# Expert weights split into high and low parts during the feed-forward stage, and the expert stage's activation low parts made on VectorE

## What is computed

```python
def _attn_ref(r, k, v, w, u):            # 4 batches, 8 heads, 768 steps, head size 48
    ...
        cur = np.einsum('bhd,bhe->bhde', u[None] * kt, vt)
        y[:, :, t] = np.einsum('bhd,bhde->bhe', rt, state + cur)
        state = w[None, :, :, None] * state + np.einsum('bhd,bhe->bhde', kt, vt)

def _moe_ref(x, w_in, w_out):            # x 3072 x 384, w_in 384 x 2048, w_out 2048 x 384
    h = x @ w_in
    g = h - np.tanh(h)
    return (g @ w_out).astype(np.float32)

def _moe2_ref(x, expert_emb, tau, w1, w2):   # 8 experts, w1 384 x 1024, w2 1024 x 384 each
    ...
    expert_idx = np.argmax(logits, axis=1)
    ...
        h = np.maximum(x[mask] @ w1[e], 0.0)
        out[mask] = gate_w[mask, None] * (h @ w2[e])
```

## Time and profile before

| | |
|---|---|
| median of 3 runs | 997.98 us (991.91 to 999.63) |
| the profiled execution | 993.31 us, of which the span of its instructions is 991.2 us |
| PE (TensorE matmul) | 918.6 us busy, 93% of the span |
| PEld (TensorE weight load) | 823.9 us, 83% |
| DVE (VectorE) | 623.7 us, 63% |
| ACT (ScalarE) | 476.8 us, 48% |
| POOL (GpSimd) | 380.1 us, 38% |
| granted TensorE clock, mean | 0.960 |

### The profile page before, as it was taken

The page is one execution under the profiler, slowest core; times in us unless marked ns, Lnnn a source line. Parts: engine busy times, 40 slices in busy tenths (PEclk is TensorE's granted clock), DMA queues, the critical chain, the costliest instruction groups (busy, mean ns, idle before and its releaser), DMA issues. The chain is left out here.

```text
span 991.2 us, 17791 instructions
## 1 busy us (share of the span) xinstructions
PE 918.6 (93%) x5314; PEld 823.9 (83%) x5315; DVE 623.7 (63%) x928; ACT 476.8 (48%) x1224; POOL 380.1 (38%) x369
## 2 busy tenths in 40 slices
PE   5999999999999999999999998787978979799995
PEld 4888887899999999999999988676967868689894
DVE  8799997998888788788888768844134041300000
ACT  3455445556556556656557452233424343254441
POOL 8689992000000000000000003777576575665652
PEclk7999999999999999999999997998989898899998
DMA  7698882001000000000000013754042231001100
GB/s 210 188 258 247 249 248 75 1 2 64 1 33 32 0 32 32 0 32 32 0 0 33 1 35 143 247 188 161 32 152 84 106 119 66 31 29 47 37 12 1
DMA packets 51766, 80.74 MB, mean 81 GB/s; under 512 B 6187, under 2 KB 36045, under 8 KB 51728
## 3 DMA queue, kind: packets, MB, share of 16 engines
q1 hardware_dynamic: 37776, 64.71, 20.9%
q0 software_dynamic: 3968, 10.82, 3.3%
q10 hardware_dynamic: 9984, 4.72, 1.7%
HBM read 66.07 MB, written 15.53 MB: 82 GB/s over the span
## 5 line engine op out<-in xcount | busy, mean ns | idle before, releaser
L1028 POOL MEMSET w_l<- 128x128 f32 x1 | 0.2, 204 | 435.5 <-POOLq L632 435.5
L751 ACT ACTIVATE usq<-h_ps 128x512 f32<-128x512 f32 x96 | 57.5, 599 | 163.1 <-PE h_ps L630 163.1
L628 PE MATMUL y_ps<-wout_h,g_h 128*128 128x384 f32 x384 | 129.6, 337 | 0.3 <-DVE g_l L850 0.3
L630 PE MATMUL y_ps<-wout_h,g_l 128*128 128x384 f32 x384 | 129.3, 337 | 0.0
L629 PE MATMUL y_ps<-wout_l,g_h 128*128 128x384 f32 x384 | 129.1, 336 | 0.0
L1278 DVE CAST w_h<-w_raw 128x3072 fp32r<-128x3072 f32 x14 | 34.9, 2491 | 138.9 <-PE e_bank L1350 134.2
L1321 POOL TENSOR_TENSOR ex_hT_l<-ex_hT,ex_hT_h 128x512 fp32r<-128x512 f32 x62 | 98.8, 1615 | 59.8 <-ACT ex_hT_h L1442 59.8
L1348 PE MATMUL e_bank<-w_h,ex_xT_h 128*128 x186 | 82.5, 444 | 39.5 <-POOL ex_xT_l L1311 35.6
L628 PE MATMUL h_ps<-xT_h,win_h 128*128 (+1 forms) x288 | 115.7, 402 | 0.8 <-DVE diff L843 0.8
L630 PE MATMUL h_ps<-xT_h,win_l 128*128 (+1 forms) x288 | 113.6, 394 | 0.0
L629 PE MATMUL h_ps<-xT_l,win_h 128*128 (+1 forms) x288 | 113.3, 394 | 0.0
(11 more groups left out here) (205 smaller groups left out, 2240.2 us busy)
## 6 DMA issues: line engine op xcount, KB each, us to landing
w_raw<-in_w SPq DMA_DIRECT2D x16, 1536.0 KB, 7.0
rT_sb<-in_rT SPq DMA_DIRECT2D x48, 96.0 KB, 2.6
kT_sb<-in_kT SPq DMA_DIRECT2D x48, 96.0 KB, 2.8
k_sb<-in_k SPq DMA_DIRECT2D x24, 192.0 KB, 2.9
r_sb<-in_r SPq DMA_DIRECT2D x24, 192.0 KB, 3.1
v_sb<-in_v SPq DMA_DIRECT2D x24, 192.0 KB, 3.5
x_dram<-xt_sb ACTq DMA_DIRECT2D x48, 96.0 KB, 3.2
xg_sb<-x_dram SPq DMA_DIRECT2D x6, 768.0 KB, 4.7
```

The costliest lines, as they stand in the source:

```text
L628: pe.matmul(out, lh, rh, start=start, stop=False)
L630: return pe.matmul(out, ll, rh, start=False, stop=stop)
L751: act.activation(usq[:, f % 2, :], h_ps[f % 2][:, :], ACT.Square).then_inc(u_done, 1)
```

## The change

The splitting of the expert weights leaves the expert stage. In every step of the feed-forward stage one piece of 128 x 512 of the 96 pieces of `w1` and `w2` is loaded (`load_piece`), its high part is made by ScalarE (`piece_high`, after `high`), its low part by GpSimd (`low` of the gpsimd block), and both are stored to two scratch tensors in DRAM, `w12_h` and `w12_l` (`store_piece`). The raw pieces have four buffers (`SPARE`), the parts two each (`MADE`). In the expert stage SyncE loads both parts of an expert straight into the slots, 6 MB in four transfers, and passes on that they have landed (`pass_turn`), after the transfers of turns 0 to 2 are issued. `w_raw` and all splits of it are gone. The low parts of the activations are now made by VectorE, which takes the transposed block from PSUM; ScalarE's plain copies `xT` and `hT` are gone, and so are GpSimd's subtractions. The host lays the raw weights out by piece.

```diff
@@ -637,14 +655,33 @@
                         sp.wait_ge(y_copied, B * g + b + 1)
                         sp.dma_start(x2_tiles[b, g], x2_sb[:, b, :]).then_inc(x2_stored, 16)
 
+                def load_piece(g, f):
+                    s = f % SPARE
+                    sp.dma_start(ew_raw[:, s, :], piece_of(w12, g, f)).then_inc(ew_loaded[s], 16)
+
+                def store_piece(g, f):
+                    s = f % MADE
+                    sp.wait_ge(ew_h_made, KF * g + f + 1)
+                    sp.dma_start(piece_of(w12_h, g, f), ew_h[:, s, :].bitcast(F32)).then_inc(ew_h_stored[s], 16)
+                    sp.wait_ge(ew_l_made, KF * g + f + 1)
+                    sp.dma_start(piece_of(w12_l, g, f), ew_l[:, s, :].bitcast(F32)).then_inc(ew_l_stored[s], 16)
+
                 def group(g, last):
                     if not last:
 
                         sp.wait_ge(xT_l_made, KD * g + KD)
                         load_group(sp, g + 1)
-                    if not isinstance(g, int) or last:
-                        store(g - 1)
-
+                    for f in range(KF):
+                        store_piece(g, f)
+                        if f + SPARE < KF:
+                            load_piece(g, f + SPARE)
+                        elif not last:
+                            load_piece(g + 1, f + SPARE - KF)
+                        if f == LAG and (not isinstance(g, int) or last):
+                            store(g - 1)
+
+                for f in range(SPARE):
+                    load_piece(0, f)
                 sp.dma_start(small[:, 0:1], tau.to_broadcast([P, 1])).then_inc(tau_in, 16)
 
...
@@ -652,6 +689,24 @@
                 groups(sp, group)
                 store(CH - 1)
                 sp.wait_ge(x2_stored, 16 * NT)
+                for i in range(MADE):
+                    sp.wait_ge(ew_h_stored[i], 16 * CH * KF // MADE)
+                    sp.wait_ge(ew_l_stored[i], 16 * CH * KF // MADE)
+
+            @block.gpsimd
+            def _(pool):
+                def low(g, f):
+                    s = f % MADE
+                    wait_apart(pool, passed_pool, (ew_h_made, KF * g + f + 1),
+                               (ew_l_stored[s], 16 * (KF // MADE * g + f // MADE)))
+                    pool.tensor_tensor(ew_l[:, s, :], ew_raw[:, f % SPARE, :], ew_h[:, s, :].bitcast(F32),
+                                       ALU.subtract).then_inc(ew_l_made, 1)
+
+                def group(g, last):
+                    for f in range(KF):
+                        low(g, f)
+
+                groups(pool, group)
 
             @block.tensor
...
@@ -762,6 +817,13 @@
                     wait(act, g_used, n - RING + 1)
                     act.activation(g_h[:, f % RING, :], poly[:, f % RING, :], ACT.Copy).then_inc(gh_done, 1)
 
+                def piece_high(g, f):
+                    s = f % MADE
+                    wait_apart(act, passed_x, (ew_loaded[f % SPARE], 16 * (TURNS * g + f // SPARE + 1)),
+                               (ew_h_stored[s], 16 * (KF // MADE * g + f // MADE)),
+                               (ew_l_made, KF * g + f + 1 - MADE))
+                    act.activation(ew_h[:, s, :], ew_raw[:, f % SPARE, :], ACT.Copy).then_inc(ew_h_made, 1)
+
                 def finish(g, b):
                     act.wait_ge(y_done, B * g + b + 1)
...
@@ -802,6 +864,7 @@
                         quads(n0 + f, f)
                         if f >= 1 or has_last:
                             high(n0 + f - 1, (f - 1) % KF)
+                        piece_high(g, f)
                         if has_last and f == LAG - 1:
                             for b in range(B):
...
@@ -933,22 +995,28 @@
         turn_of = sb("turn_of", [1, ST], I32)
         last_tile = sb("last_tile", [1, E], I32)
         banks = [psum(f"e_bank{i}", [P, 512]) for i in range(8)]
-        w_in_raw = [sem(f"w_in_raw{part}") for part in range(PARTS)]
-        first_high = sem("first_high")
-        w_high = sem("w_high")
-        w_split = sem("w_split")
+        w_loaded = [[sem(f"w_loaded{slot}_{part}") for part in range(PARTS)] for slot in range(SLOTS)]
+        w_ready = sem("w_ready")
+        NP = WIDE // PIECE
 
         def load_turn(eng, turn):
 
+            slot = turn % SLOTS
             e = eng.value_load(expert_of[0:1, turn:turn + 1], min_val=0, max_val=E - 1) if turn else 0
+            if turn >= SLOTS:
+                ends = eng.value_load(last_tile[0:1, turn - SLOTS:turn - SLOTS + 1], min_val=0, max_val=ST)
+                eng.wait_ge(tile_done, ends + 1)
             for part in range(PARTS):
-                wait(eng, w_split, PARTS * (turn - 1) + part + 1)
-                eng.dma_start(w_raw[:, part, :].rearrange("p (a f) -> p a f", a=(KD, KE)[part]),
-                              (w1, w2)[part][bass.ds(e, 1)].rearrange("o (a p) f -> p (o a) f", p=P)
-                              ).then_inc(w_in_raw[part], 16)
-
-        def part_of(x, turn, part):
-            return x[:, turn % SLOTS, part * WIDE:(part + 1) * WIDE]
+                for x, src in ((w_h, w12_h), (w_l, w12_l)):
+                    eng.dma_start(x[:, slot, part * WIDE:(part + 1) * WIDE].bitcast(F32).rearrange("p (a f) -> p a f", a=NP),
+                                  src[bass.ds((e * PARTS + part) * NP, NP)].rearrange("a p f -> p a f")
+                                  ).then_inc(w_loaded[slot][part], 16)
+
+        def pass_turn(eng, turn):
+
+            for part in range(PARTS):
+                eng.wait_ge(w_loaded[turn % SLOTS][part], 2 * 16 * (turn // SLOTS + 1))
+                eng.sem_inc(w_ready, 1)
...
@@ -1058,10 +1126,6 @@
             act.wait_ge(r_dve, 8)
             act.activation(ex[:, :, :], eq[:, :, :], ACT.Exp).then_inc(r_act, 1)
 
-            for part in range(PARTS):
-                act.wait_ge(w_in_raw[part], 16)
-                act.activation(part_of(w_h, 0, part), w_raw[:, part, :], ACT.Copy).then_inc(first_high, 1)
-
         def route_tensor(pe):
             keep_warm(pe, banks[7], ident, 8)
...
@@ -1256,29 +1318,35 @@
                 load_turn(sp, 0)
 
                 sp.wait_ge(tables_made, 3)
-                for turn in range(1, E):
+                sp.wait_ge(rows_made, 2)
+                for turn in range(1, SLOTS):
                     load_turn(sp, turn)
+                for turn in range(SLOTS):
+                    pass_turn(sp, turn)
+                for turn in range(SLOTS, E):
+                    load_turn(sp, turn)
+                    pass_turn(sp, turn)
 
             @block.vector
             def _(dve):
                 route_vector(dve)
 
-                for part in range(PARTS):
-                    dve.wait_ge(first_high, part + 1)
-                    dve.tensor_tensor(part_of(w_l, 0, part), w_raw[:, part, :],
-                                      part_of(w_h, 0, part).bitcast(F32), ALU.subtract).then_inc(w_split, 1)
-
-                for turn in range(1, E):
-                    if turn >= SLOTS:
-
-                        ends = dve.value_load(last_tile[0:1, turn - SLOTS:turn - SLOTS + 1], min_val=0, max_val=ST)
-                        dve.wait_ge(tile_done, ends + 1)
-                    for part in range(PARTS):
-                        dve.wait_ge(w_in_raw[part], 16 * (turn + 1))
-                        dve.tensor_copy(part_of(w_h, turn, part), w_raw[:, part, :]).then_inc(w_high, 1)
-                        dve.wait_ge(w_high, PARTS * (turn - 1) + part + 1)
-                        dve.tensor_tensor(part_of(w_l, turn, part), w_raw[:, part, :],
-                                          part_of(w_h, turn, part).bitcast(F32), ALU.subtract).then_inc(w_split, 1)
+                def x_low(i, j, k):
+                    s = k % 2
+                    dve.wait_ge(xT_high, i + 1)
+                    dve.tensor_tensor(xT_l[:, s, :], t_ps[:, 0:DM], xT_h[:, s, :].bitcast(F32),
+                                      ALU.subtract).then_inc(xT_split, 1)
+
+                def tile(i, j, k):
+                    if not is_last(i):
+                        x_low(*later(i, j, k, 1))
+                    for hf in range(2):
+                        dve.wait_ge(hT_high, 2 * i + hf + 1)
+                        dve.tensor_tensor(hT_l[:, hf, :], hT_ps[hf][:, :], hT_h[:, hf, :].bitcast(F32),
+                                          ALU.subtract).then_inc(hT_split, 1)
+
+                x_low(0, 0, 0)
+                loop(dve, tile)
 
             @block.gpsimd
...
@@ -1305,21 +1373,9 @@
                                             o_sb[:, s, :], None, bounds_check=ALL - 1,
                                             oob_is_err=False).then_inc(scattered[s], 16)
 
-                def x_low(i, j, k):
-                    s = k % 2
-                    pool.wait_ge(xT_high, i + 1)
-                    pool.tensor_tensor(xT_l[:, s, :], xT[:, s, :], xT_h[:, s, :].bitcast(F32),
-                                       ALU.subtract).then_inc(xT_split, 1)
-
                 def tile(i, j, k):
```

(30 more changed lines are left out.)

33 lines of the change are left out of this document (20 added, 13 removed).

## The result

The changed kernel takes **1002.23 us** (median of 14 runs, 997.12 to 1003.9); the kernel before took 994.97 in the same sessions (14 runs, 991.91 to 1000.94). So it is 0.6% slower, within the 1% named in the prediction, and 22 us above the 980 forecast.

The account below looks back on a forecast made before the run. TensorE bounds feed-forward, with VectorE close behind and becoming the bound after the change. Terms: -56.2 (experts) - 2 (last tile) + 40 (feed-forward) = -18, from a median of 997.98 to 980 us, own range 968 to 993.

Parts of the forecast that it names:

- The start of the experts: Expert stage: first product near 622.0 us behind SyncE's eight transfers, 4.2 us in all; tile 0 takes 6.0 us.
- SyncE is held while it issues: Rival, expert start: the last issue waits for three to four transfers, some 12 us; 992 us, chance 0.10.
- The price of the lock: Feed-forward: each GpSimd subtraction takes 1.07 us from VectorE, whose step becomes 4.65 and bounds the stage; +40 us.
- The two rivals on its size (0.47 and 1.26 to 1.72): Feed-forward lock price a step: 0.47 us, total 943, chance 0.12; 1.26, total 998, 0.10; 1.72, total 1042, 0.08.
- The experts' pace: Expert stage: full pace from tile 1 on, 29 x 9.65 = 279.9 us; VectorE's low parts cost nothing.
- -2 in the last tile: End of expert stage: the wait ahead of `second` shrinks, VectorE having the first subtraction ready about 1.3 us sooner; -2 us.
- ScalarE's copy and the transfers in feed-forward: Feed-forward: one 0.64 us copy and three 256 KB transfers a step, both costed at nothing.
- TensorE's clock in feed-forward: Feed-forward: TensorE idles about 0.4 us a step but its clock stays at 1.00; nothing charged.
- Gathers late behind the weights: Rival, first expert tiles: gathers wait behind 12.6 MB of weights, two or three stops of 3 us or so; 990 us, chance 0.08.

Follow-up runs that it names:

- Experiment 1: Changed kernel with turn 0 passed on before the transfers of turns 1 and 2 are issued; 978.90 us, ratio 0.9847.
- experiment 4: Changed kernel with GpSimd's feed-forward subtraction replaced by a memset, low parts of the expert weights zero; 960.07 us (1 run).
- experiment 5: Changed kernel with GpSimd's feed-forward subtraction replaced by a copy of the raw piece, reading one SBUF operand; 961.84 us (1 run).
- experiment 2: Changed kernel with GpSimd's feed-forward subtraction also waiting for VectorE's predicated copy of the same step; 976.87 us, ratio 0.9813.
- experiment 7: Changed kernel with turn 0 passed first, GpSimd's subtraction gated on VectorE's predicated copy, and activations' low parts back on GpSimd; 958.49 us, ratio 0.9639.

## Why the prediction was wrong

The forecast was -18 us, the medians moved by +7.3 and the profiled executions by +4.2. The 980 itself stands on 997.98 for the kernel before, which 14 runs put at 994.97; the same -18 from there gives 977. By its own steps:

- **The start of the experts: the step that failed.** The prediction had the right wait in the right place ("behind SyncE's list"), but priced each of the eight issues at 0.35 us from the earlier trace rows, where transfers are of 192 KB, and summed to a first product near 622, 3.5 us sooner than before. These are 1.5 MB each: three go at 0.4 us, the others at 3 to 5. Experiment 1 measures the error at 23 us: 20.4 of gap (63.5 to 43.0) and 1.7 of the slower clock in tile 0 (8.03 against the 6.0 assumed; 6.33 once the stop is gone). The rival "SyncE is held while it issues" named this cause with a chance of 0.10, and at 12 us its price was half of the true one: it let three to four transfers be waited out, and it was five, at 3.1 to 5.4 us each. This term alone turns -18 into +4; the other misses (+2.9 in feed-forward, -2.0 at the start, -0.6 at the end) nearly cancel. With it mended (experiment 1) the kernel runs at 978.90, 16.3 us under the kernel before in the same sessions. That this lies beside the forecast's 980 is in part luck, since the baseline of the forecast was 3 us too high.
- **The price of the lock: right.** 1.07 us a step was taken from attention, 1.10 was measured; the step was forecast at 4.65 and is 4.68 to 4.70, the stage at 450.8 and is 453.8. It falls on L919, before `large`, as said, in 75 of 96 steps; that it would be `low` in the 15 with an `x_low` was not foreseen and changes little in the sum. Experiments 4 and 5 show that GpSimd's reading of SBUF is behind it; experiments 2 and 5 move and shrink it. The two rivals on its size (0.47 and 1.26 to 1.72) did not occur. The Trainium skill (SBUF — State Buffer, section Who interferes with whom) makes the shared ports an exclusive lock: whoever issues first has them for its whole instruction, and the other is blocked meanwhile. The trace agrees, with L919 ending 0.55 us after GpSimd's subtraction in the median; but the rule does not make this a loss of the whole 1.26, as the prediction read it, for some 0.3 to 0.4 us of GpSimd's instruction pass while `low` is still running, and GpSimd itself is held meanwhile (1.53 instead of 1.29). What VectorE loses is 1.10. The Trainium skill's other statement, that a GpSimd instruction which only writes does not contend with a VectorE instruction of two SBUF inputs, is what experiment 4 shows, 0.684 beside a memset.
- **The experts' pace: right.** 29 x 9.65 from tile 1 on, in every kernel of the study. VectorE's low parts end before they are asked for, except at the ends: that the second part of the change was worth only some 4 us (experiment 7) agrees with costing it at nothing in the steady pace and at -2 in the last tile, where 2.6 were measured.
- **ScalarE's copy and the transfers in feed-forward: right**, at nothing (experiment 4). TensorE's clock in feed-forward: nearly. It was to stay at full speed; it is at 0.50 for 3.4 us at three of the group boundaries, where TensorE idles for `x_sb` (L833), small against the rest.
- **Gathers late behind the weights:** not seen; tile 1 waits 0.51 us for VectorE only. The stop of 21 us gave the gathers time, but in experiment 1, without the stop, the tiles keep 9.65 from tile 1 on as well.

What the study adds: the idea of splitting in the feed-forward stage was good, and most of both losses could be avoided. With turn 0 passed on first and the split wholly on ScalarE and VectorE, the kernel runs at 0.947 of the time before.

## What to carry to other kernels

An issue of a DMA was not a fixed cost here: price it by the size of what the queue has still to send, and let a queue pass on what has landed before it issues the next long list. Work given to an idle GpSimd was not free where it read SBUF while VectorE was near the bound: compare what it takes from VectorE (1.10 us here) with what VectorE would need to do it itself (0.60). Look for slack between the two engines that bound a stage before moving work there; 0.42 a step vanished in it, 1.10 did not.

## What the runs showed of the hardware

- SyncE's queue took three transfers of 1.5 MB at 0.4 to 0.5 us each, with few exceptions, and the fourth was held in every list of every kernel here. A held issue took 2.4 to 6.3 us over all traces, about what one transfer takes by an estimate from the 387 GB/s above (1.57 MB, 4.1 us). With 0.75 MB it took six (once five). In experiment 1's trace the fourth issue ends at 668.89 and the first transfer has landed at 668.88; the later ones end within 2.2 us of the landing of the transfer three before. An issue can thus hold everything behind it on its engine.
- GpSimd beside VectorE's two-operand SBUF instruction: memset 0, copy 0.42, subtraction 1.10 us. In the changed kernel and in experiments 2 and 5 the stretched two-operand instruction ends some 0.55 us after GpSimd's, so its loss follows from when GpSimd starts and how long it takes: 0.31 + 1.53 + 0.55 after the start of `low`, instead of 0.60 + 0.68, is 1.11; 0.31 + 1.30 + 0.55 after the start of `diff`, instead of 1.28, is 0.88. `large`, with one SBUF operand, was stretched as well, from 0.41 up to 0.84 by the copy and up to 1.54 by the subtraction; `diff`, with one operand in PSUM, never (0.71 at most), though in experiment 2 GpSimd ran beside it in 95 steps; nor was GpSimd held by it (1.30 beside `diff`, 1.50 beside the two-operand `x_low`).
- GpSimd started 0.3 to 0.4 us after the VectorE instruction that followed its releaser had started (experiment 2), so released this way it fills only the rest of a 0.6 us slot of VectorE.
